# Attention before two MLP layers on one core: where P V and the transposes of P stand in TensorE's order, and which two PSUM banks they use

## What is computed

```python
scores = scale * np.matmul(q, k.transpose(0, 1, 3, 2))
thresh = np.max(scores, axis=-1, keepdims=True) - tau
scores = np.where(scores >= thresh, scores, -1000000000.0)
scores = scores - np.max(scores, axis=-1, keepdims=True)
attn = np.exp(scores)
attn = attn / (np.sum(attn, axis=-1, keepdims=True) + 1e-09)
x = np.matmul(attn, v)          # heads side by side: 2304 x 512
h = np.maximum(x @ w_in, 0.0)
x = (s * (h * h) + b) @ w_out   # first MLP
h = x @ w_in2
x = (np.maximum(h, 0.0) + alpha * np.minimum(h, 0.0)) @ w_out2
```

## Time and profile before

| | us |
|---|---|
| median of three runs | 1121.0 (1120.95 to 1124.82) |
| the profiled execution | 1120.8 |
| its span, first to last instruction | 1119.0 |
| first score tile of pair 2 | 48.95 |
| first score tile of pair 15, the last | 282.50 |
| last score tile of pair 15 | 295.62 |
| first matmul of the MLP | 311.27 |

### The profile page before, as it was taken

The page is one execution under the profiler, slowest core; times in us unless marked ns, Lnnn a source line. Parts: engine busy times, 40 slices in busy tenths (PEclk is TensorE's granted clock), DMA queues, the critical chain, the costliest instruction groups (busy, mean ns, idle before and its releaser), DMA issues.

```text
span 1119.0 us, 19062 instructions
## 1 busy us (share of the span) xinstructions
PE 1102.4 (99%) x5844; PEld 889.2 (79%) x5844; DVE 525.0 (47%) x1008; ACT 516.3 (46%) x942; POOL 262.9 (23%) x440
## 2 busy tenths in 40 slices
PE   8999999999999999999999999899999999999998
PEld 6677777777678888888888889788888888888897
DVE  6888888888643342242242236622332332332242
ACT  4787877878754332232232236633333333333343
POOL 2656565665654400000000008600000000000000
PEclk9999999999999999999999999999999999999999
DMA  7666665655111100000000005300100000010010
GB/s 159 163 157 152 145 145 141 147 140 128 50 47 48 47 10 0 0 0 0 0 0 0 0 5 156 104 1 1 38 0 0 1 37 0 0 37 0 0 38 19
DMA packets 86550, 59.22 MB, mean 53 GB/s; under 512 B 49376, under 2 KB 69872, under 8 KB 86512
## 3 DMA queue, kind: packets, MB, share of 16 engines
q1 hardware_dynamic: 84112, 58.17, 20.4%
q10 hardware_dynamic: 2400, 0.59, 0.3%
HBM read 30.94 MB, written 4.72 MB: 32 GB/s over the span
## 4 chain that ended last, share of the span: by engine, by line
PE 93%; SPq 3%; issue 1%; ACT 1%; DVE 1%; POOL 0%; DMA 0%; POOLq 0%; ACTq 0%; DVEq 0%
PE psum L850 24%; PE psum L848 24%; PE psum L849 24%; PE psum L966 6%; PE psum L935 5%; PE psum L877 3%; PE psum L879 3%; SPq L380 2%; PE psum L858 1%; PE psum L961 1%; PE psum L943 1%; PE psum L932 1%; SPq L344 0%; PE psum L862 0%; PE psum L971 0%
## 5 line engine op out<-in xcount | busy, mean ns | idle before, releaser
L848 PE MATMUL psum<-x_hi,win_hi 128*128 128x512 f32 (+1 forms) x640 | 238.3, 372 | 1.4 <-DVE x_lo L779 1.4
L850 PE MATMUL psum<-x_hi,win_lo 128*128 128x512 f32 (+1 forms) x640 | 238.7, 373 | 0.0
L849 PE MATMUL psum<-x_lo,win_hi 128*128 128x512 f32 (+1 forms) x640 | 238.2, 372 | 0.0
L848 PEld LDWEIGHTS psum<-x_hi,win_hi 128*128 128x128 f32 x640 | 120.3, 188 | 25.3 <-DVE x_lo L779 2.5
L849 PEld LDWEIGHTS psum<-x_lo,win_hi 128*128 128x128 f32 x640 | 120.2, 188 | 23.9
L850 PEld LDWEIGHTS psum<-x_hi,win_lo 128*128 128x128 f32 x640 | 120.2, 188 | 23.0
L797 DVE SCALAR_TENSOR_TENSOR act_r<-act_n,nalpha,act_r 128x512 f32<-128x512 f32 (+1 forms) x80 | 55.9, 698 | 158.9 <-ACT act_r L650 158.6
L721 DVE TENSOR_REDUCE negm<-psum 128x1 f32<-128x576 f32 x144 | 108.1, 751 | 35.3 <-PE psum L879 31.6
L786 DVE SCALAR_TENSOR_TENSOR act_r<-act_r,s_c 128x512 f32<-128x512 f32 (+1 forms) x80 | 69.1, 864 | 116.9 <-ACT act_r L639 116.9
L513 POOL TENSOR_SCALAR ex<-ex,none_in,rinv 128x576 f32<-128x576 f32 x144 | 118.9, 827 | 20.3 <-DVE rinv L740 18.7
L642 ACT ACTIVATE g_hi<-act_r,b_c 128x512 fp32r<-128x512 f32 (+1 forms) x80 | 54.5, 682 | 148.5 <-PE psum L850 124.3
(11 more groups left out here) (92 smaller groups left out, 1632.8 us busy)
## 6 DMA issues: line engine op xcount, KB each, us to landing
k_twice<-k_hi SPq DMA_DIRECT2D x64, 144.0 KB, 2.5
stage<-in_moe_w_out_dram SPq DMA_DIRECT2D x32, 256.0 KB, 2.7
out_dram<-stage SPq DMA_DIRECT2D x18, 256.0 KB, 2.2
q_both<-q_hi SPq DMA_DIRECT2D x32, 128.0 KB, 2.3
q_both<-q_lo SPq DMA_DIRECT2D x32, 128.0 KB, 2.3
raw_v<-in_v_dram SPq DMA_DIRECT2D x16, 256.0 KB, 2.7
win_raw<-in_moe_w_in_dram SPq DMA_DIRECT2D x16, 256.0 KB, 2.9
stage<-in_moe_w_in_dram SPq DMA_DIRECT2D x16, 256.0 KB, 2.7
```

Of the source, the lines that this page charges most:

```text
L848: nc.tensor.matmul(dst, lhs[0], rhs[0], start=first, stop=False)
L849: nc.tensor.matmul(dst, lhs[0], rhs[1], start=False, stop=False)
L850: return nc.tensor.matmul(dst, lhs[1], rhs[0], start=False, stop=final)
```

## The change

- Transposes (L935, L932) and P V no longer have a bank each. Banks 6 and 7 are used in rotation by everything that was in either (`shared`). A run (one group of transposes, or one whole P V group) waits for the copy of the run two before it (`wait_for_bank`); before, a transpose waited for the copy of the transpose just before it.
- Each P V group is done without interruption, ten matmul instructions, group 0 in step 16 and group 1 in step 20. The transposes stand in steps 8 to 14.
- K stands at place 3, between tiles 1 and 2. Before, it stood at place 5.
- Both output copies are in ScalarE's step 20. ScalarE does the exponential first in a step, then output copies, copies of transposes, and the high part of q or k.
- `split_x(0, 0)` moves from step 29 to step 32 of the drain, where the output copies stand too.
- In the opening ScalarE's queue issues k of pair 0; SyncE's queue issues q of 0, tau, and q and k of 1. SyncE stacks pair 0 before it loads q of pair 2. `run_idle` makes three transposes, not five.

```diff
-        LAYOUT = ["Q", 0, 1, 2, 3, "K", "L", 4, 5, 6, 7, 8]
+        LAYOUT = ["Q", 0, 1, "K", 2, 3, "L", 4, 5, 6, 7, 8]
-        TURNS = [(5, 0, False), (7, 1, False), (8, 2, False), (9, 3, False), (10, 0, True),
-                 (12, 4, False), (13, 5, False), (14, 6, False), (15, 7, False), (16, 4, True)]
+        TURNS = [(8, 0, False), (9, 1, False), (10, 2, False), (10, 3, False), (11, 0, True),
+                 (11, 4, False), (12, 5, False), (13, 6, False), (13, 7, False), (14, 4, True)]
-        PV = {13: [(0, 0), (0, 1)], 15: [(0, 2), (0, 3)], 16: [(0, 4)],
-              20: [(1, 0), (1, 1)], 22: [(1, 2), (1, 3)], 23: [(1, 4)]}
+        PV = {16: [(0, 0), (0, 1), (0, 2), (0, 3), (0, 4)], 20: [(1, 0), (1, 1), (1, 2), (1, 3), (1, 4)],
+              }
-        FIRST_OUT, SECOND_OUT = 16, 23
+        FIRST_OUT, SECOND_OUT = 20, 20
...
-            load_qk(0, 0)
+            load_raw_q(sp, 0, 0)
             sp.dma_start(tau_c[:], tau.partition_broadcast(P)).then_inc(tau_in, DMA)
+            load_raw_q(sp, 1, 1)
+            load_raw_k(sp, 1, 1)
+            stack(0, 0)
             sp.wait_ge(filled, 1)
             load_raw_q(sp, 2, 0)
-            stack(0, 0)
...
+                if after.tile:
+                    exp(after)
                 for group, at in ((0, FIRST_OUT), (1, SECOND_OUT)):
...
-                if after.tile:
-                    exp(after)
+                for turn in turns_at(n0, l):
+                    copy_turned(turn)
                 if later.prepares:
                     qk_high(later)
-                for turn in turns_at(n0, l):
-                    copy_turned(turn)
...
-                if m == FIRST_OUT - POS + 1:
+                if m == min(FIRST_OUT + 1, SECOND_OUT) - POS:
                     split_x(0, 0)
-            load_raw_q(act, 1, 1)
-            load_raw_k(act, 1, 1)
+            load_raw_k(act, 0, 0)
...
+            def wait_for_bank(n, kind, which):
+                back, kind, which = two_runs_back(kind, which)
+                if static(n) and n + back < 0:
+                    return
+                if kind == "turn":
+                    wait(pe, turned_out, (n + back) * TURNS_PP + which + 1)
+                else:
+                    wait_alone(pe, o_out, 2 * (n + back) + which + 1)
...
-                    run_idle(5)
+                    run_idle(3)
```

## The result

The changed kernel takes 1122.7 us (median of twelve, 1120.9 to 1124.8), the kernel before 1121.0 beside it (twelve, 1119.4 to 1124.8). The ratio is 1.0017, with a 95% interval of 1.0009 to 1.0025: slower by 1 to 3 us, inside 0.5%. Forecast were 1123.0 us and a range of 1116 to 1128.5. The profiled execution took 1121.9 us, with a span of 1120.1.

The account below looks back on a forecast made before the run. TensorE, busy 1102.4 of 1119.0 us, was taken as the bound, SyncE's transfers in the opening. Terms 0.75 - 5.5 + 1.2 + 3.85 = +0.3, plus 1.7 for the clock, put 1121.0 at 1123.0 us; range 1116 to 1128.5.

Parts of the forecast that it names:

- The pair: One attention pair: 18.02 us less 0.70 for visits and 0.62 for old waits, plus 0.90 new waits, gives 17.60.
- Pair 2 to pair 15: From pair 2's first tile to pair 15's: 233.55 us falls to 228.05, -5.5 us, including 0.6 off after pair 2's wait.
- The opening: Up to pair 2's first tile: SyncE's 60 transfers end later, TensorE waits some 2 us for `k_twice`; +0.75 us.
- First tile to tile 8 of pair 15: Last pair: 13.12 us becomes 14.35, because a whole group 1 P V precedes tiles 7 and 8; +1.2 us.
- The drain: Tile 8 of the last pair to the MLP: 15.65 us becomes 19.5, with splits ahead of last scaling; +3.85 us.
- the clock: Holes before pair 2, in the drain and ahead of the MLP may lower it; one of three counted, +1.7 us.
- (b): Rival: the clock is lowered at all three holes, 1126.5 us; chance 0.10.
- (c): Rival: long P V visits starve VectorE more, a pair stays at 18.02 us, total 1128.5 us; chance 0.13.
- (d): Rival: VectorE and ScalarE chain is looser, waits 0.2 us a pair, pair 16.9, total 1113.9 us; chance 0.12.
- (e): Rival: switch cost lies in operand kinds, not P V visits; pair 17.60 + 0.70, total 1132.1 us; chance 0.04.
- (f): Rival: pauses lower the clock in every pair, 24.5 us, total 1147.5 us; chance 0.02.
- (a): Rival: no lowered clock anywhere, 1121.3 us; chance 0.20.

Follow-up runs that it names:

- e1: Changed kernel with each P V group cut in two visits again; 1129.14 us, ratio 1.0073 to the kernel before.
- e7: Changed kernel with the loads and five idle transposes of the old opening; 1123.75 us, ratio 1.0030 to the kernel before.
- e3: Changed kernel with the split of the first MLP tokens three steps earlier in the drain; 1120.76 us, ratio 1.0001 to the kernel before.
- e4: Changed kernel with ScalarE's and GpSimd's weight splits three steps later in the drain; 1120.68 us, ratio 0.9999 to the kernel before.
- e5: Changed kernel with both the token split three steps earlier and the weight splits three steps later; 1116.89 us, ratio 0.9970 to the kernel before.
- e11: Changed kernel with twenty useless transposes in the drain's hole ahead of tile 7's transposes; 1123.46 us, ratio 1.0022 to the kernel before.
- e6: Kernel before with ScalarE's and GpSimd's weight splits three steps later in the drain; 1120.94 us, ratio 1.0002 to the kernel before.
- e10: Changed kernel with five idle transposes in each of the first steps instead of three, loads as changed; 1123.08 us, ratio 1.0023 to the kernel before.
- e12: Changed kernel with q and k of pair 2 loaded before v of pair 0, constants and first weights after the stacking; 1119.00 us, ratio 0.9989 to before.
- e8: Changed kernel with K back at place 5, between tile 3 and L; 1128.03 us, ratio 1.0069 to the kernel before.
- e9: Changed kernel with the edits of both e5 (drain) and e12 (opening loads); 1113.54 us, ratio 0.9939 to the kernel before.

## Why the prediction was right, and where it was not

**Luck in the sum.** The median, 1122.7 us, lies 0.3 us from the forecast. That is closer than the terms were: they were off by 0.4 to 1.1 us each, both ways. What held is the mechanism of the two large ones, the gain in the pair and the loss in the drain.

**The pair, 17.60: measured 17.61, but two terms were off and cancelled.** TensorE's own work is 16.93 us, not 16.70: of the 0.70 saved, 0.47 shows. The visits cost what the earlier trace rows said (2.30, entry 0.22 for 0.13). In the 0.70 I had left the tail chunks out. They now stand directly behind the 64-column matmuls. This is the kernel before, TensorE in order of time, group 0's tail chunk:

```profile
200.82 0.60 PE L961 MATMUL psum<-pt_tails,raw_v_tail 128*128 128x256 f32 x2
201.25 0.82 PE L943 MATMUL psum<-ident,ex 128*128 128x128 f32 x6
```

0.43 us then, 198.09 - 197.55 = 0.54 now, and 0.11 more in group 1 as well: 0.22 of the 0.23. The waits are 0.68 us, not 0.90: q 0.21 (forecast 0.20), tile 4's transposes 0.19 (0.22), tile 6 0.27 (0.32), and the wait for the mask of tile 1 is 0.01 in place of 0.16. The Trainium skill ("TensorEngine Tiling (Array Packing)", section "Key Properties") says that a change of tiling mode drains the engine. The traces show a price, 0.20 us for a visit in e1's group 0 and 0.35 by the rows of before; that a drain is what costs it, no run here shows.

**Pair 2 to pair 15, -5.5: measured 277.95 - 49.03 = 228.92, -4.6.** The 0.6 us that I took off for "everything is in hand behind the wait at pair 2" did not come. The missing wait is not the reason: e7, which does wait there for 1.52 us, took 277.83 - 48.93 = 228.90.

**The opening, +0.75: measured +0.08 in the profiled execution, for another reason.** TensorE did not wait 2 us for `k_twice` at pair 2 in it. I had looked at SyncE's last transfer and not at one in the middle. TensorE reaches k of pair 2 at 29.55 us (32.37 - 2.82), where the kernel before took it at 36.05, and its transfers are issued at 27.9 us in both. The last `k_twice` ended at 45.68 us, not 47.6: 60 transfers took 38.6 us (0.643 each), where they took 40.2 before.

But this is one execution. e3, e4, e5 and e11 have the changed kernel's instructions up to the drain, and their pair 2 starts at 49.54, 48.42, 50.73 and 49.84 us; of the old opening there are 48.95 and 48.59 (e6). All five of the new opening wait for k of pair 2 (0.88 to 3.36 us), and what follows decides. In e5 the clock is 0.66 between 30 and 40 us, and TensorE itself comes late. In e11 it is 1.00, TensorE comes early and waits 2.18 us for `k_twice`: the case that I had forecast, near the 49.7 us forecast, with the lowered clock behind it. The middle one of the five is 49.54, 0.8 us behind the mean of the two old ones: the forecast's +0.75, but by few executions.

**First tile to tile 8 of pair 15, +1.2: measured 292.64 - 277.95 = 14.69, +1.6.** At 281.78 us TensorE waits 0.76 us for GpSimd's scaling, a wait that the prediction doesn't name.

**The drain, +3.85, and the clock, +1.7: measured +5.1 together.** Step by step, from tile 8's scores: tile 7 scaled at 8.4 us (forecast 8.3), second `win_lo` done at 11.6 (11.5), tile 8 scaled at 12.4 (12.4), its copies done at 15.6 (14.4), P V's copy from 19.0 (17.6), MLP at 20.8 (19.5). Of the error of 1.3 us, 1.1 is P V of group 0 at the low clock (with the hole filled, e11 has 19.67), and that is the clock term, sized 1.7 and put in one of three places. e4, e3 and e11 price the drain: 3.7 us for the early weight splits, 1.1 of them the clock, and 1.8 for the tokens. The hole ahead of the MLP left the clock at 1.00; the hole at pair 2 did not arise in this execution, but the clock fell in the opening before it.

**The MLP, 0: measured -1.06.** The prediction kept its 807.7 us without a reason. e10 ties the difference to the idle transposes, and the rows to one transfer of weights. Without it the span would have grown by 2.2 us, not 1.1.

Sum of the measured: 0.08 - 4.6 + 1.6 + 5.1 - 1.1 = +1.1 us of span, against +2.0. The medians differ by 1.75.

**The rivals.** (b) fell in the profiled execution: one hole of three lowered the clock. (c) fell: the pair did not stay at 18.02. (d) fell: 0.68 us of waits, not 0.2. (e) fell by the pair's 17.61 and by e1. (f) fell: the clock is 1.00 in the pairs, with 0.68 us of waits each. Between the forecast and (a) the difference is how often the clock falls, and that varies from execution to execution.

**Open.** In which stretches the clock fell in the executions that were not profiled. In the changed kernel's profiled one, the stretches below 1.00 in the opening (10 to 40 us) and the drain (300 to 310) make up the whole of its mean of 0.994. The clock was 0.66 to 0.75 between 20 and 30 us in the changed kernel, e1, e5, e11 and e12, and 0.94 or more in e3, e4, e7, e8, e9 and e10. e9's five executions (1113.0 to 1114.3) spread least. What ScalarE's new order within a step is worth by itself was not tried.

## What to carry to other kernels

A gain in the steady part is easily given back at the two ends, where the same instructions meet other neighbours: this order wins 4.6 us between pair 2 and pair 15 and loses 6.7 us in the last pair and drain, and three small moves of work at the ends make it 6.6 us faster than the kernel before (e9). When work moves forward, follow every transfer that it will then ask for, not only the last one. Instructions without use in a hole kept the clock up behind it in the one trace of e11, but the median was no better; taking the holes away (e5, e9) lowered the median. And a difference of under 1 us at one place, read from one execution of each kernel, may be no difference: the start of pair 2 varied by 2.3 us over five executions with the same instructions up to there.

## What the runs showed of the hardware

- The clock after a hole: 2.59 us without work ahead of 301.14, then a clock of 0.71 and a P V of 3.45 us for 1.95; with 20 transposes in the hole 1.00 and 1.95. The 1.80 us ahead of 313.43 left it at 1.00. In e1, where the clock had been 0.50 between 310 and 315 us, it fell again, to 0.70, behind the 1.80 us ahead of 320.96. The Trainium skill ("TensorE: Matmul & The Clock Gate", section "HAM oscillation — how this bites in real kernels") tells of a kernel whose clock fell behind each wait for its data. The wait here is for another engine, and e11 agrees in kind.
- Executions of one kernel can differ by 4 to 5 us with their mean granted clock (e4: 1117.4 at 1.000, 1122.1 at 0.992), so one profile of a small edit at the ends can show 3.7 us where the medians show 1.4.
- Eighteen idle transposes more in the first steps (5844 matmuls for 5826) go with an MLP that takes 1.06 us longer at one place some 680 us later, in all four kernels that had them. There ScalarE takes up a piece of weights 3.30 to 3.34 us behind its issue, having waited for it, where the changed kernel takes it up after 2.70 us without a wait.
